# Attention's q, k and stacks: laid out beforehand and written in place by engines

## The reference

```python
def _attn_ref(q, k, v, proj):                      # q, k, v: (2, 8, 768, 64), proj: (64, 6)
    q_bits = (np.einsum('bhsd,dk->bhsk', q, proj) > 0).astype(np.int64)
    k_bits = (np.einsum('bhsd,dk->bhsk', k, proj) > 0).astype(np.int64)
    q_bucket = np.sum(q_bits * powers, axis=-1)
    k_bucket = np.sum(k_bits * powers, axis=-1)
    mask = q_bucket[:, :, :, None] == k_bucket[:, :, None, :]
    scores = scale * np.matmul(q, k.transpose(0, 1, 3, 2))
    scores = np.where(mask, scores, -1000000000.0)
    scores = scores - np.max(scores, axis=-1, keepdims=True)
    attn = np.exp(scores)
    attn = attn / (np.sum(attn, axis=-1, keepdims=True) + 1e-09)
    return np.matmul(attn, v).astype(np.float32)
```

## Time and profile before

| | |
|---|---|
| median of 3 runs | 492.6 us (491.82 to 494.3) |
| the profiled execution, its own time | 493.54 us |
| its span, first to last instruction | 491.8 us |
| PE busy | 456.3 us (93%) |
| DVE busy | 304.9 us (62%) |
| ACT busy | 227.4 us (46%) |
| POOL busy | 109.0 us (22%) |
| attention | from 0 to about 271 us |
| experts and last stage | to the end |

### The profile page before, as it was taken

The page is one execution under the profiler, slowest core; times in us unless marked ns, Lnnn a source line. Parts: engine busy times, 40 slices in busy tenths (PEclk is TensorE's granted clock), DMA queues, the critical chain, the costliest instruction groups (busy, mean ns, idle before and its releaser), DMA issues.

```text
span 491.8 us, 8308 instructions
## 1 busy us (share of the span) xinstructions
PE 456.3 (93%) x2817; PEld 333.8 (68%) x2817; DVE 304.9 (62%) x582; ACT 227.4 (46%) x476; POOL 109.0 (22%) x194
## 2 busy tenths in 40 slices
PE   2889999999999999999699979976999999999997
PEld 1677678777777876777476634332788888888885
DVE  3467778777787777787454241014998486648661
ACT  1366667866677766678455421113634131122110
POOL 4224354443454343444211000000000000000000
PEclk9989999999999999999979979997799999999999
DMA  6446677667667667773954739999000020001002
GB/s 148 125 106 206 178 201 219 200 202 216 174 205 218 189 209 192 197 206 94 262 177 161 270 115 370 398 407 335 1 0 2 0 87 0 1 35 51 1 0 85
DMA packets 55831, 76.74 MB, mean 156 GB/s; under 512 B 29312, under 2 KB 33280, under 8 KB 55296
## 3 DMA queue, kind: packets, MB, share of 16 engines
q1 hardware_dynamic: 55808, 76.44, 50.0%
HBM read 51.45 MB, written 3.15 MB: 111 GB/s over the span
## 4 chain that ended last, share of the span: by engine, by line
PE 84%; DMA 8%; DVE 2%; SPq 2%; ACT 2%; issue 1%; ACTq 0%; DVEq 0%
PE ps L649 16%; PE ps L669 12%; PE ps L659 12%; PE ps L895 9%; PE ps L897 9%; PE ps L896 9%; DMA ring_lo<-in_moe_w 4%; DMA stack_a<-low 2%; PE ps L633 2%; PE ps L625 2%; PE ps L876 2%; PE ps L803 2%; PE ps L822 2%; PE ps L734 1%; PE ps L863 1%; SPq L433 1%
## 5 line engine op out<-in xcount | busy, mean ns | idle before, releaser
L1029 DVE TENSOR_REDUCE max_raw<-ps 128x1 f32<-128x768 f32 x96 | 91.9, 957 | 56.9 <-PE ps L649 55.8
L649 PE MATMUL ps<-stack_b,stack_a 96*128 96x384 f32 (+1 forms) x384 | 96.1, 374 | 9.4 <-DMA stack_a<-low 7.1
L916 ACT ACTIVATE arena<-ps,neg_max 128x768 f32<-128x768 f32 x96 | 86.8, 904 | 17.4 <-DVE neg_max L1032 16.0
L910 ACT COPY arena<-ps 128x384 f32<-128x384 f32 x144 | 64.6, 482 | 57.2 <-PE ps L659 57.1
L649 PEld LDWEIGHTS ps<-stack_b,stack_a 96*128 96x128 f32 (+1 forms) x384 | 65.6, 197 | 33.7 <-issue 18.7
L659 PE MATMUL ps<-ident,arena 128*128 128x128 f32 x576 | 81.3, 277 | 1.1 <-ACT arena L910 1.0
L895 PE MATMUL ps<-w_high,g_high 128*128 128x512 f32 x192 | 75.8, 395 | 2.3 <-DVE g_low L1210 2.3
L896 PE MATMUL ps<-w_low,g_high 128*128 128x512 f32 x192 | 75.7, 394 | 0.0
L897 PE MATMUL ps<-w_high,g_low 128*128 128x512 f32 x192 | 75.6, 394 | 0.0
L659 PEld LDWEIGHTS ps<-ident,arena 128*128 128x128 f32 x576 | 70.3, 143 | 5.1 <-ACT arena L916 1.4
L669 PE MATMUL ps<-arena 128*64 128x384 f32 x384 | 68.0, 491 | 0.0
(11 more groups left out here) (119 smaller groups left out, 437.1 us busy)
## 6 DMA issues: line engine op xcount, KB each, us to landing
ring_lo<-in_moe_w SPq DMA_DIRECT2D x12, 1024.0 KB, 5.5
ring_lo<-in_moe_w SPq DMA_DIRECT2D x6, 2048.0 KB, 13.7
stack_a<-high SPq DMA_DIRECT2D x32, 192.0 KB, 3.2
stack_b<-high SPq DMA_DIRECT2D x32, 192.0 KB, 3.3
arena<-in_moe_w SPq DMA_DIRECT2D x3, 2048.0 KB, 8.5
arena<-in_q SPq DMA_DIRECT2D x16, 192.0 KB, 3.1
arena<-in_k SPq DMA_DIRECT2D x16, 192.0 KB, 3.4
arena<-in_v SPq DMA_DIRECT2D x16, 192.0 KB, 2.4
```

The lines of the kernel that those rows point to most:

```text
L649: last = nc.tensor.matmul(s_ps[p % 2][:, c, :], a[r][0:used, rows], b[r][0:used, cols], start=(a is stack_a1), stop=(a is stack_a2))
L910: nc.scalar.copy(probs_t[:, place(r, p), b * HALF:(b + 1) * HALF, :], ring[b].rearrange("p (a s) -> p a s", a=HALF)).then_inc(t_taken[b], 1)
L916: nc.scalar.activation(probs[:, p % 2, :].rearrange("p (c s) -> p c s", c=2), s_ps[p % 2], ACT.Exp, bias=neg_max[:, r, p:p + 1], scale=SCA ...
L1029: nc.vector.tensor_reduce(max_raw[:, r, p:p + 1], s_ps[p % 2], axis=AX.XY, op=ALU.max)\
```

## The change

`kernel()` now lays q and k out before the launch (`laid_out`): turned, with tile columns in order, and each twice, so that both halves of the 128 partitions hold the 64 dimensions. The program loads 128 rows of 3 KB for each of q and k. Constants (the identity, the stacked identity, the projections, per-row scales) come in one small DMA instead of being made by POOL.

`turn_qk`, `take_qk`, `place_high` and `place_low` are gone. In the steady loop POOL writes the stacks in place with five instructions for each head, from `both` (q and k as loaded) by per-partition scales 1 or -1/8. The bits are written by DVE as before, then scaled by POOL in place (`scale_bits`), and only they are copied by DMAs. For head 0 and 1 ACT, DVE and POOL share this.

The scores carry the scale and a minus sign now, so the smallest is the row's best. The mask rows give zero where the buckets agree. Empty rows are told by a smallest score of at least `EMPTY`: then `exp_scale` and `exp_bias` are both 0, every exponential is 1, and the row becomes the mean of v by itself. `exp_scale` and `exp_bias` take the place of `neg_max`, and the sum of v, `e_recip` and `finish` are gone. PE runs some matmuls on ones ahead of the first scores (`warm`).

```diff
-        high = rounded("high", arena_at, [P, S])
...
+        both = part(2 * S).rearrange("p (w s) -> p w s", w=2)
...
-            def load_qk(m, r, dst):
...
+            def load_qk(n, r, dst):
+                for w in range(2):
+                    sp.dma_start(dst[:, w, :], qk_dram[bass.ds(n * 2 + w, 1), :, :].rearrange("a p s -> p (a s)"))\
                         .then_inc(qk_in[r], DMA)
-            def load_v(m, r):
+            def load_v(n, r):
                 sp.dma_start(nat_v[:, r, :, :].rearrange("p t d -> p (t d)"),
-                             v_dram[bass.ds(m, 1), :, :].rearrange("a (p t) d -> p (a t d)", p=P))\
...
             def place_bits(n, r):
-                sp.wait_ge(hash_taken, n + 1)
+                sp.wait_ge(bits_scaled, n)
                 for j in range(NQ):
                     sp.dma_start((stack_a2, stack_b2)[j % 2][r][D:D + QUAD, (j // 2) * HC:(j // 2 + 1) * HC].bitcast(F32),
                                  bits[j * QUAD:(j + 1) * QUAD, :].bitcast(F32)).then_inc(bits_in[r], DMA)
-            def place_high(n, r):
...
-            load_qk(0, 0, nat)
...
+            sp.dma_start(both[:, 0, :], qk_dram[0]).then_inc(qk_in[0], DMA)
+            sp.dma_start(const[:, :], consts).then_inc(consts_in, DMA)
+            load_qk(1, 1, both_second)
+            sp.wait_ge(hash_ready, 1)
+            sp.wait_ge(q_low, 1)
+            sp.wait_ge(k_low, 1)
+            sp.wait_ge(k_again, 1)
+            load_qk(2, 0, both)
...
             def body(m, r, k):
+                if within(m, 2) and (not isinstance(m, int) or m > 0):
+                    sp.wait_ge(hash_ready, m + 2)
+                    sp.wait_ge(k_again, m + 2)
+                    load_qk(m + 2, r, both)
                 if within(m, 1):
                     place_bits(m + 1, 1 - r)
-                    place_low(m + 1, 1 - r, low)
                     if not isinstance(m, int) or m > 0:
                         sp.wait_ge(o_ready, m)
                     load_v(m + 1, 1 - r)
                 if not isinstance(m, int):
                     fill_half(1 - r, k + r - 1)
-                if within(m, 3):
...
                 if isinstance(m, int) and m == HEADS - 3:
                     fill(sp, 6)
                 elif isinstance(m, int) and m == HEADS - 2:
                     sp.wait_ge(scores_ready, (HEADS - 1) * TILES)
-                    sp.wait_ge(high_in[1], PAIRS * 4 * DMA)
-                    sp.wait_ge(low_in[1], PAIRS * 2 * DMA)
...
-            def split_high_of(n, r, k):
...
+            nc.gpsimd.memset(ones[:, :], 1.0).then_inc(ones_set, 1)
+            lower, upper = slice(0, D), slice(D, P)
+            over = lambda column, rows: column[rows, :].broadcast_to([D if rows != slice(0, P) else P, S])
+            def low_q(n, r, src):
+                pool.wait_ge(q_high, n + 1)
+                nc.gpsimd.tensor_tensor(stack_a2[r][lower, :], src[lower, 0, :], stack_a1[r][lower, :], ALU.subtract)\
+                    .then_inc(q_low, 1)
+            def high_k(r, src):
+                nc.gpsimd.tensor_tensor(stack_b1[r][:, :], src[:, 1, :], over(k_scale, slice(0, P)), ALU.mult)\
+                    .then_inc(k_high, 1)
+            def low_k(n, r, src):
+                pool.wait_ge(k_high, n + 1)
+                nc.gpsimd.tensor_tensor(stack_b1[r][upper, :], src[upper, 1, :], stack_b1[r][upper, :], ALU.subtract)\
+                    .then_inc(k_low, 1)
+            def scale_bits(n):
+                pool.wait_ge(k_low, n + 1)
+                pool.wait_ge(hash_taken, n + 1)
+                nc.gpsimd.tensor_tensor(bits[:, :], bits[:, :], bit_times.broadcast_to([P, HC]), ALU.mult)\
+                    .then_inc(bits_scaled, 1)
+            pool.wait_ge(consts_in, DMA)
+            pool.wait_ge(qk_in[0], 2 * DMA)
+            low_q(0, 0, both)
+            pool.wait_ge(qk_in[1], 2 * DMA)
+            pool.wait_ge(k_low, 1)
+            high_k(1, both_second)
+            low_k(1, 1, both_second)
+            low_q(1, 1, both_second)
             def body(m, r, k):
                 if within(m, 1):
-                    split_low_of(m + 1)
...
+                    scale_bits(m + 1)
                 if within(m, 2):
-                    if not isinstance(m, int) or m > 0:
-                        pool.wait_ge(x_done, m + K0)
-                    split_high_of(m + 2, r, k + r + 1)
+                    pool.wait_ge(qk_in[r], (k + 2) * 2 * DMA)
+                    pool.wait_ge(scores_ready, m * TILES + TILES)
+                    nc.gpsimd.tensor_tensor(stack_a1[r][:, :], both[:, 0, :], over(q_scale, slice(0, P)), ALU.mult)\
+                        .then_inc(q_high, 1)
+                    high_k(r, both)
+                    low_q(m + 2, r, both)
+                    low_k(m + 2, r, both)
+                    nc.gpsimd.tensor_tensor(stack_b2[r][lower, :], both[lower, 1, :], over(k_scale, lower), ALU.mult)\
+                        .then_inc(k_again, 1)
             heads(pool, body)
...
-            def turn_qk(n, r, k, src):
...
+            def warm(count):
+                for _ in range(count):
+                    nc.tensor.matmul(ps[:, 3, 0:P], ones[:, :], ones[:, :], start=True, stop=True)
+            def hashes(src):
+                for j in range(NQ):
+                    last = nc.tensor.matmul(hash_ps[j * QUAD:(j + 1) * QUAD, :], proj_w,
+                                            src[:, j % 2, (j // 2) * HC:(j // 2 + 1) * HC], start=True, stop=True)
                 last.then_inc(hash_ready, 1)
-            def sum_v(m, r):
...
             def scores(m, r, p):
...
                     last = nc.tensor.transpose(o_ps[:, t * P:(t + 1) * P], o_t[:, j * P:(j + 1) * P], ident[:, :])
                 last.then_inc(o_back, 1)
-            pe.wait_ge(ident_ready, 1)
...
+            pe.wait_ge(ones_set, 1)
+            warm(7)
+            pe.wait_ge(consts_in, DMA)
+            pe.wait_ge(qk_in[0], 2 * DMA)
+            hashes(both)
+            warm(5)
             pe.wait_ge(hash_taken, 1)
-            turn_qk(1, 1, 0, nat_second)
-            pe.wait_ge(high_in[0], 4 * DMA)
-            pe.wait_ge(low_in[0], 2 * DMA)
+            pe.wait_ge(qk_in[1], 2 * DMA)
+            hashes(both_second)
+            pe.wait_ge(q_low, 1)
+            pe.wait_ge(k_low, 1)
+            pe.wait_ge(k_again, 1)
+            pe.wait_ge(first_bits, 1)
             scores(0, 0, 0)
             scores(0, 0, 1)
...
                     if p == TILES - 2 and within(m, 1):
-                        pe.wait_ge(high_in[1 - r], (k + r + 1) * 4 * DMA)
-                        pe.wait_ge(low_in[1 - r], (k + r + 1) * 2 * DMA)
+                        pe.wait_ge(q_low, m + 2)
+                        pe.wait_ge(k_low, m + 2)
+                        pe.wait_ge(k_again, m + 2)
                         pe.wait_ge(bits_in[1 - r], (k + 1) * NQ * DMA)
                     pe.wait_ge(probs_ready, m * TILES + p + 1)
                     if p + 2 < TILES or within(m, 1):
                         scores(*target(m, r, k, p))
-                    if p == TILES - 2 and within(m, 2):
...
                     transpose_probs(m, p)
                     if p == 0 and within(m, 1):
                         if not isinstance(m, int) or m > 0:
-                            pe.wait_ge(sum_taken, m)
-                        hashes(m + 1)
+                            pe.wait_ge(qk_in[1 - r], (k + r + 1) * 2 * DMA)
+                            pe.wait_ge(hash_taken, m + 1)
+                            hashes(both)
+                    if p == 0 and within(m, -1):
+                        pe.wait_ge(v_in[1 - r], (k + r) * DMA)
                     if p < 2 and within(m, -1):
                         times_v(m - 1, 1 - r, p)
                     if p == 2 and within(m, -1):
                         transpose_o(m - 1, 1 - r)
-                    if p == TILES - 1:
-                        sum_v(m, r)
+                    if p == TILES - 1 and within(m, -1):
+                        pe.wait_ge(x_scaled, m)
...
             def exps(m, r, p):
                 g = m * TILES + p
-                act.wait_ge(max_ready, g + 1)
+                act.wait_ge(min_ready, g + 1)
                 nc.scalar.activation(probs[:, p % 2, :].rearrange("p (c s) -> p c s", c=2), s_ps[p % 2], ACT.Exp,
-                                     bias=neg_max[:, r, p:p + 1], scale=SCALE,
+                                     bias=exp_bias[:, r, p:p + 1], scale=exp_scale[:, r, p:p + 1],
                                      accum_out=row_sum[:, r, p:p + 1]).then_inc(probs_ready, 1)
...
+            act.dma_start(both[:, 1, :], qk_dram[1]).then_inc(qk_in[0], DMA)
+            act.dma_start(nat_v[:, 0, :, :].rearrange("p t d -> p (t d)"), v_dram[0]).then_inc(v_in[0], DMA)
+            act.wait_ge(ones_set, 1)
+            nc.scalar.activation(denom[:, 0:1], ones[:, 0:1], ACT.Exp)
+            act.wait_ge(consts_in, DMA)
+            act.wait_ge(qk_in[0], 2 * DMA)
```

(97 more changed lines are left out.)

244 lines of the change are left out of this document (37 added, 207 removed).

## The result

The changed kernel takes 514.1 us (median of 4 runs, 511.2 to 515.2) against 493.3 for the kernel before beside it: ratio 1.042, 95% interval 1.036 to 1.047. It is slower by some 21 us where I had forecast 12.3 less. The profiled execution took 513.2, its span is 511.4 against 491.8: 19.6 more, and this is what the traces have to account for.

A forecast was written before the change was run, and what follows sets the result against it. PE was taken as the bound (84% of the chain of waits), its steps 2 to 5 only filling a loop through DVE and ACT. Terms -7.0 - 1.3 + 2.6 - 4.8 - 1.8 = -12.3 gave 480 us against the median; range 470 to 507.

The forecast's parts named there:

- If DVE gets in there, ACT decides: Inside a head: DVE's exp_bias goes before POOL's difference, so the next head's scores start at 7.0; 15.2 us a head, chance 0.42.
- rival 2: Inside a head: POOL starts its 1.82 us difference first and DVE waits; 17.0 us a head, 505 us; chance 0.30.
- the start: Up to head 1's first scores: they start at 23 instead of 30.04 us, -7.0 (-4 to -9).
- rival 4: At the start: placings of bits alternate with POOL's instructions; 4 us worse, 484, inside the forecast's range; no chance of its own.
- steps 2 to 5: Last four of a head's six steps, a loop through DVE and ACT: 7.03 us before the change, 7.0 forecast with the hold.
- steps 0 and 1: First two of a head's six steps, with the hash and the product with v: some 7.95 us of PE work.
- the 0.15 that I had added for a delay in step 0: In a head's step 0: exp_bias waiting for a difference delays DVE's copy and PE's transposes by 0.15 us.
- I take 12: Head 0's first scores: at 12 us, between 10.7 and 15.7, against 14.84 before the change.
- Rival 1: Inside a head: exp_bias is not held by POOL; 14.65 us a head, 472 to 473 us; chance 0.20.
- That the bits come in time: Each head's bits: landing at 16.8, wanted at 18.5, covered by 1.7 us; late bits or a like wait had chance 0.08.
- That the weights' transfer no longer stands before head 15: Head 15's period: the 2 MB transfer is issued earlier, right behind load_v(14), and 20.0 us becomes 15.2, -4.8.
- The half speed behind it: After head 15's wait: PE's half speed goes, 5.6 us from 246.30 to 251.92 become about 3.8, -1.8.

## Why the prediction was wrong

**The step that failed** is "If DVE gets in there, ACT decides (4.28 + 1.66: exponential 5.93, S(0) 7.0)", the choice between two orders, to which I gave 0.42 against 0.30. I had seen the place, the 0.1 us in which it is decided, and both prices: 15.2 us a head or 17.0. Measured are 16.8, and 17.05 over the 13 periods with the two falls of the clock. The argument against, "nothing but that the walk puts DVE there as often before as after", treated each head as a new draw. The run with `exp_bias` first shows that it is none: the first hold lines both engines up at POOL's end, and the rest of the head is the same sum of durations each time. From the common end at 164.55 POOL starts `low_q` 1.39 later, one product less the 0.08 by which its instructions overlap, and DVE `exp_bias` 1.45 later (a copy, a reduction, `exp_scale`). Both parts could be had from the trace of the kernel before. The rows named in the prediction show no two POOL instructions in a row, but its timeline does, and it has the next `neg_max` behind the earlier trace rows:

```profile
136.06 1.01 POOL L592 TENSOR_TENSOR x_sb<-x_sb,arena 128x384 f32 x1 [4.18 <-DVE x_sb L1087]
137.03 0.32 POOL L576 TENSOR_TENSOR v_part<-arena 128x64 f32<-128x64 f32 x1
...
168.29 0.15 DVE L1032 TENSOR_SCALAR neg_max<-max_raw 128x1 f32<-128x1 f32 x1
```

POOL's second instruction starts 0.04 before the first ends. Two such overlaps make 1.39 of a product of 1.47. DVE's `neg_max` at 168.29 starts 1.40 after the one before has ended (166.89), and with one small instruction more that is 1.47. So POOL comes first by 0.08, as one choice for all heads, and rival 2 was likelier than the forecast by these sums. A range over the whole of it would still have missed: its 505, with 5.1 for the start and 2.8 for the clock below, makes 513, and rival 4 stood in the prediction only beside the forecast's own 480.

**Where the order goes the other way the forecast holds.** The kernel with the memset has the changed kernel's work and holds, but for the order, and its head takes 15.2 us, the figure of the forecast. That it fits to 0.1 is partly luck: steps 2 to 5 take 7.13 us against my 7.0 and steps 0 and 1 take 8.07 against 7.95, for the reasons under "Too small", while the 0.15 that I had added for a delay in step 0 did not come: that step is no longer than with the one-input `exp_bias` (4.42 against 4.43). With the start mended too it would be at 486.8 - 5.8 = 481, an estimate from two runs; the forecast was 480.

**The start** (-7.0, measured -1.9) is the second term that failed. "I take 12" for the first scores lay between 10.7, if DVE gets at SBUF at each end of POOL's, and 15.7, if it lets one by each time. It lets one by, and before the first placing two: 14.88. Rival 4 was the case too, and some 5 us of the miss are its. It is a choice of the same kind as in the heads, and I had costed the two apart, as if they were independent.

**Too small**: the exponential with a scale from SBUF, 0.99 and not 0.90, about 0.17 a head where nothing is held (6.88 against 6.71); step 0 with the new hash, 0.2 a head. Rival 1's 14.65 became 14.9 to 15.1 by these two. The clock's falls in two heads, 2.8 us, were in no term. Of the 1.4 at the end the slot sums have 0.7 (5.20 us for 24 matmuls against 4.52) and the wait for the experts' transfer 0.3. Over these matmuls the granted clock was 0.54 against 0.62, which accounts for the 0.7 (5.20 x 0.54 and 4.52 x 0.62 are both 2.8); why the clock was lower there is open.

**Right**: that `exp_bias` is held and `exp_scale` is not, and that it is the second input that does it. That half-size differences on POOL cost what whole ones do (1.82, against the bound of 0.91). That the bits come in time: they land in 2.4 to 2.5 us, and no head waits for them. That the weights' transfer no longer stands before head 15: it was issued at 246.35, behind the bits, and PE doesn't wait; the period fell by 3.1 and not 4.8 only because it has a held `exp_bias` like the others. The half speed behind it went, -1.8 as forecast. I had expected that transfer before 225; it comes where the longer heads put it.

## What to carry to other kernels

A DVE instruction with two SBUF inputs in a loop that limits the kernel can be held for a whole instruction of POOL's, however small it is (1.77 us for one column here): look for a form with one tensor input, here the second one as a per-partition scalar. Where such a pair is left, don't count the order as a matter of chance: add up what each engine does from the last common end to the next start, and where the two sums lie within 0.1 us, take the worse, or put something between. Check an expected gain for the part that the old kernel can have alone, as the weights' transfer here.

## What the runs showed of the hardware that I had not expected

- `exp_bias` as a `tensor_scalar` whose second scalar comes from an SBUF column was not held in any of 96 beside the same POOL work: 200 to 207 ns. It takes 0.05 us more than with two tensor inputs and no hold (0.15).
- Here the two engines stay in step once one has waited for the other: the gap of 0.06 to 0.07 us came back in 12 of 14 heads, and again with DVE's two small instructions exchanged.
- A placing of bits on DVE that waited while POOL went from one instruction to the next without a gap (8.92 to 8.88 by the profile's ends) was not let in between. Where POOL's next came 0.07 to 0.08 after the last, for which it waits (10.34 to 10.41, 12.21 to 12.29), the waiting placing was done 0.2 after the end. A missing gap alone does not decide it: in the heads a held `exp_bias` was done at 164.56, with POOL's next instruction begun at 164.51 and the one before over at 164.55. No run tests what does.
- A difference of 64 partitions by 768 columns on POOL takes 1.82 us, as the one of 128 partitions before.
- The exponential of 128x768 takes 992 ns with its scale in SBUF and 901 with a constant.
- After 1.6 us of idle PE the granted clock fell in two of 14 heads of the changed kernel. It fell in two, two and three heads of the three kernels that keep the long hold (the first bits earlier, the constant scale, `exp_bias` first), and between 28 and 268 us in none of the five without it. So the falls, 1.4 us each, are part of the hold's price. Why in these heads, and not in the others with the same wait, stays open.
